# A fused attention and mixture-of-experts kernel: the first expert block outside the loop, expert weights loaded further ahead and split in another order, scatters counted per buffer

## The chip, the cores and the metric

The kernel runs on one core of a Trainium2 chip. The metric is the time of the whole program on the device in microseconds (us). Three runs of the kernel before gave 707.31, 708.02 and 710.58; the median is 708.02. TensorE, VectorE, ScalarE and GpSimd are also written PE, DVE, ACT and POOL; SP is the engine that issues most transfers.

## The reference

Three stages follow one another. The arrays are float32.

```python
# 1: linear attention, B=4, H=8, S=768, D=48
cur = einsum('bhd,bhe->bhde', u[None] * kt, vt)
y[:, :, t] = einsum('bhd,bhde->bhe', rt, state + cur)
state = w[None, :, :, None] * state + einsum('bhd,bhe->bhde', kt, vt)
# 2: dense MLP over 3072 tokens, 384 -> 2048 -> 384
h = x @ w_in
z = maximum(0.01 * h, h) @ w_out
# 3: top-1 mixture of 8 experts (384 -> 1024 -> 384) with a skip score
do_compute = z @ w_skip > 0
e_idx = argmax(z @ w_gate); gate_w = softmax(z @ w_gate)[e_idx]
out = z + gate_w * (maximum(z @ w1[e_idx], 0) @ w2[e_idx])   # only where do_compute
```

## The kernel before, in words

**Everything up to the experts.** Attention runs in 24 chunks of 128 tokens, the MLP in 8 groups of three chunks and 16 steps each, 128 steps in all (STEPS). Every float32 product is made of three float32r products: a value is split into a high part (ScalarE's copy, `_hi`) and a low part (VectorE's difference, `_lo`), and hi·hi, hi·lo and lo·hi are summed. The results z go to `z_rows` in memory and to `out`. Token numbers are scattered by expert into `id_list`, which comes back as `found`; the last group's are placed by TensorE products while the MLP ends (`place_last`, L1405 on). The rows of the first expert block come from two places: `zg_early` (GpSimd's gather, L1758, turned by TensorE, L827) and the last group's rows straight from `z_sb` (L836). Behind L827 TensorE ranks the last group (L751, L753), VectorE's `slot` (L1413) waits for that, and the first block's rows wait for what follows it.

**The expert blocks.** Tokens of one expert are worked on in blocks of 128; a block belongs to one expert. How many blocks there are and which expert each has is known at run time only, in `plan`; TensorE, ScalarE, VectorE and GpSimd each run a loop of eight rounds with four blocks in a round (UNROLL), with a branch around each block, and read from `plan` with register loads (`value_load`). In block j:

- TensorE turns the hidden rows of block j (L855, `hidden_turned`), makes the first product of block j+1 (L816, 18 matmuls, w1), turns the gathered rows of block j+2 (L808, `turn_rows`), and makes the second product of block j (L911, 24 matmuls, w2).
- ScalarE copies the turned hidden rows to `eht_hi` (L1158), and, where block j is the first of its expert e, w2 of expert e+1 to `w2_hi` in three pieces (L1130); then ReLU on the hidden rows of block j+1 (L1137, L1138), `zt_hi` for block j+2 (L1133), and last, where block j+1 is the first of its expert e, w1 of expert e+1 to `w1_hi` in three pieces (L1037).
- VectorE does the low parts in the same order: `eht_lo` (L1634), w2 (L1647), `zt_lo` (L1577), w1 (L1663), and then `res` (L1670), the gate times the second product plus the row itself.
- GpSimd takes the token numbers (`put` L1787, `get` L1792), waits for `res`, gathers the rows of block j+4 (`zg`, four buffers, L1740) and scatters `res` of block j to `out` (L1799). It begins a block only when the scatter of the block before has landed: all scatters count on one semaphore `s_rows_out`. `res` and `put` have two buffers each.

Each engine works through its own list in the order written; the order is set by hand. Raw weights have two places per matrix (expert number even or odd). SP loads them (`load_w1` L521, `load_w2` L529; each is two transfers of 768 KB) and tells ScalarE with `report`. w1 of experts 0 and 1 is loaded and split during the MLP's last group (L1043, L1339), w2 of expert 0 is loaded at the end of the MLP. For each further expert SP waits until the place is free, loads w1, waits again, loads w2, and waits for both to land before it goes on:

```python
report(0)
report(1)
for e in range(2, E):
    if e == 2:
        sp.wait_ge(rows_in[0], 16)
    sp.wait_ge(s_w1_lo, PIECES * (e - 1))
    load_w1(e)
    sp.wait_ge(s_w2_lo, PIECES * (e - 1))
    load_w2(e)
    report(e)
```

Ahead of its loop TensorE makes block 0's first product, turns block 1's rows and block 0's hidden rows, and multiplies out the gate table (`list_gates`, L849).

## Time and profile before

| | |
|---|---|
| time, median of 3 runs | 708.02 us |
| the profiled execution's own time | 704.92 us |
| its span, first to last instruction | 703.0 us |
| mean granted clock of TensorE | 0.992 of full speed |
| TensorE matmuls | 676.8 us busy, 96% of the span |
| VectorE | 411.4 us, 59% |
| ScalarE | 306.6 us, 44% |
| GpSimd | 90.9 us, 13% |
| DMA | 78.04 MB, mean 111 GB/s |
| expert stage in the trace | from about 547 us to 696 us, 14 blocks |

Busy times are of single engines and overlap. In rows of the timeline the first number is the start in us from the span's start, the second how long the row's instructions last; "[1.79 <-issue]" is idle time of that engine just before and what ended it, where "issue" is time in which nothing is seen to be waited for (register loads, branches, dispatch). Starts of neighbouring matmuls overlap by up to 0.25 us, since their ends are modelled. The waits of an engine that is not on the path cost nothing.

### The profile page before, as it was taken

To read this page: it belongs to the slowest core of one execution; us is meant where nothing else is said; L and a number is where in the kernel's file an instruction comes from. 1 tells how busy PE (TensorE), PEld (TensorE's weight loads), DVE (VectorE), ACT (ScalarE), POOL (GpSimd) and SP (SyncE) were. 2 spreads that over 40 slices of the span, in tenths; PEclk is the share of its full clock that TensorE was granted. 3 is DMA by queue.
4 is the path that set the end of the run, shared out by engine and by line. 5 is a ranking of instruction groups with operands and counts; after the bars stand their busy time and mean duration, and the time that the engine had idled before them with its cause. 6 is when DMAs were issued, how large, how long until landed. Compare 5 with 4: busy or idle time off the path is not lost.

```text
span 703.0 us, 14162 instructions
## 1 busy us (share of the span) xinstructions
PE 676.8 (96%) x4374; PEld 643.2 (91%) x4375; DVE 411.4 (59%) x859; ACT 306.6 (44%) x665; POOL 90.9 (13%) x115
## 2 busy tenths in 40 slices
PE   8989999999999999999999999999999889999993
PEld 7989999999999999999999999999998678898883
DVE  8775656655655565556555554633476781573851
ACT  4545435433434443354334344433354362654750
POOL 6530000100010001001000100010020311423411
PEclk9999999999999999999999999999999999999997
DMA  8826624211422132242114222004304586382600
GB/s 242 275 88 202 202 69 136 68 37 38 132 67 69 48 99 62 64 135 68 40 34 132 68 69 73 30 11 168 116 11 159 157 321 233 98 308 74 210 20 8
DMA packets 39081, 78.04 MB, mean 111 GB/s; under 512 B 8578, under 2 KB 27299, under 8 KB 39024
## 3 DMA queue, kind: packets, MB, share of 16 engines
q1 hardware_dynamic: 34064, 62.96, 28.7%
q10 hardware_dynamic: 2432, 9.76, 3.7%
q0 software_dynamic: 2528, 4.60, 2.1%
q8 instruction: 32, 0.52, 0.3%
q14 instruction: 25, 0.20, 0.1%
HBM read 61.29 MB, written 13.00 MB: 106 GB/s over the span
## 4 chain that ended last, share of the span: by engine, by line
PE 83%; DMA 5%; DVE 4%; issue 3%; ACT 1%; DVEq 1%; POOL 1%; ACTq 0%; POOLq 0%; SPq 0%
PE bank L723 29%; PE bank L741 28%; PE bank L816 5%; PE bank L911 5%; PE bank L605 4%; PE bank L661 3%; PE bank L656 3%; PE bank L674 2%; DMA raw<-in_experts 2%; PE bank L699 1%; DMA zg<-z_rows,get 1%; DMA out<-res,put 1%; PE bank L855 1%; PE bank L643 1%; DVE w_lo L1663 1%
## 5 line engine op out<-in xcount | busy, mean ns | idle before, releaser
L1006 ACT ACTIVATE h_sb<-bank 128x384 f32<-128x384 f32 x128 | 62.9, 492 | 246.8 <-PE bank L723 246.8
L1293 DVE TENSOR_TENSOR h_sb<-h_sb,bank 128x384 f32<-128x384 f32 x128 | 70.8, 553 | 169.1 <-ACT h_sb L1006 168.6
L723 PE MATMUL bank<-x_hi,win_hi 128*128 128x384 f32 x384 | 134.7, 351 | 2.0 <-DVE win_lo L1315 1.9
L741 PE MATMUL bank<-wout_hi,g_hi 128*128 128x394 f32 x384 | 132.0, 344 | 0.0
L741 PE MATMUL bank<-wout_hi,g_lo 128*128 128x394 f32 x384 | 131.7, 343 | 0.0
L741 PE MATMUL bank<-wout_lo,g_hi 128*128 128x394 f32 x384 | 131.6, 343 | 0.0
L723 PE MATMUL bank<-x_hi,win_lo 128*128 128x384 f32 x384 | 129.4, 337 | 0.0
L723 PE MATMUL bank<-x_lo,win_hi 128*128 128x384 f32 x384 | 129.3, 337 | 0.0
L1300 DVE TENSOR_TENSOR g_lo<-h_sb,g_hi 128x384 fp32r<-128x384 f32 x128 | 72.0, 563 | 32.7 <-ACT g_hi L1013 31.7
L1013 ACT ACTIVATE g_hi<-h_sb 128x384 fp32r<-128x384 f32 x128 | 66.6, 521 | 43.6 <-DVE h_sb L1293 41.2
L723 PEld LDWEIGHTS bank<-x_hi,win_hi 128*128 128x128 f32 x384 | 72.2, 188 | 8.6 <-issue 6.2
L1705 POOL DMA_INDIRECT id_list<-idgate,dst x21 | 21.3, 1014 | 446.3 <-DVE dst L1398 442.0
L741 PEld LDWEIGHTS bank<-wout_hi,g_lo 128*128 128x128 f32 x384 | 72.8, 190 | 0.0
L741 PEld LDWEIGHTS bank<-wout_lo,g_hi 128*128 128x128 f32 x384 | 72.6, 189 | 0.0
L741 PEld LDWEIGHTS bank<-wout_hi,g_hi 128*128 128x128 f32 x384 | 72.5, 189 | 0.0
L723 PEld LDWEIGHTS bank<-x_lo,win_hi 128*128 128x128 f32 x384 | 72.4, 189 | 0.0
L723 PEld LDWEIGHTS bank<-x_hi,win_lo 128*128 128x128 f32 x384 | 72.2, 188 | 0.0
L963 ACT ACTIVATE am<-const,diag 128x128 f32<-128x128 f32 x168 | 53.2, 391 | 0.0
L911 PE MATMUL bank<-w_hi,eht_hi 128*128 x112 | 38.8, 346 | 3.8 <-DVE eht_lo L1634 3.3
L911 PE MATMUL bank<-w_hi,eht_lo 128*128 x112 | 37.5, 335 | 0.0
L911 PE MATMUL bank<-w_lo,eht_hi 128*128 x112 | 37.5, 335 | 0.0
L1250 DVE COPY_PREDICATED am<-const,bank 128x512 f32<-128x512 uint32 x48 | 32.8, 739 | 2.1 <-PE bank L605 1.4
(217 smaller groups left out, 964.1 us busy)
## 6 DMA issues: line engine op xcount, KB each, us to landing
raw<-in_experts SPq DMA_DIRECT2D x32, 768.0 KB, 6.1
rkt<-in_rk_t SPq DMA_DIRECT2D x46, 192.0 KB, 3.6
rkn<-in_rk_nat SPq DMA_DIRECT2D x21, 384.0 KB, 4.1
z_rows<-z_sb SPq DMA_DIRECT2D x27, 192.0 KB, 2.7
v<-in_v_nat SPq DMA_DIRECT2D x24, 192.0 KB, 2.9
out<-z_sb SPq DMA_DIRECT2D x24, 192.0 KB, 2.8
stage<-in_win ACTq DMA_DIRECT2D x4, 768.0 KB, 4.4
stage<-in_wout_t ACTq DMA_DIRECT2D x4, 768.0 KB, 6.1
```

Source lines behind the costliest of these rows:

```text
L605: mm = pe.matmul(scores_in(n)[q][:, P * p:P * p + P], kb[n % 2][rows, p, :], rt[n % 2][rows, p, :], start=True, stop=True)
L723: mm = pe.matmul(h_ps[t % 2][:, 0:GT], a[:, kk, cols], b[G % 2][:, kk, :], start=n == 0, stop=n == 3 * KT - 1)
L741: mm = pe.matmul(z_ps[i][:, 0:ZW], a[t % 3][:, tok], b[:, f, :], start=f == 0 and j == 0, stop=f == FT - 1 and j == 2)
L816: mm = pe.matmul(eh_ps[c][:], a[par][:, kk, :], b[:, bass.ds(base + EF * kk + 512 * c, 512)], start=kk == 0 and a is zt_hi and b is w1_hi, ...
L911: mm = pe.matmul(ey_ps[u % 2][:, 0:DM], a[:, f, :], b[:, bass.ds(odd * EW + DM * f, DM)], start=f == 0 and a is eht_hi and b is w2_hi, sto ...
L963: ins = act.activation(am_of(n)[h % 2][:, h // 2, :], ident, ACT.Copy, scale=diag_of(n)[:, h:h + 1])
L1006: act.activation(h_sb[t % 2][:], h_ps[t % 2][:, 0:GT], ACT.Copy, scale=SLOPE).then_inc(s_h_scaled, 1)
L1013: act.activation(g_hi[t % 3][:], h_sb[t % 2][:], ACT.Copy).then_inc(s_g_hi_done, 1)
L1250: dve.copy_predicated(am_of(n)[q][:], spread(before.bitcast(U32), 1, [P, PAIRS, P]), scores_in(n)[q][:].rearrange("a (p t) -> a p t", p=PA ...
L1293: dve.tensor_tensor(h_sb[t % 2][:], h_sb[t % 2][:], h_ps[t % 2][:, 0:GT], ALU.max).then_inc(s_leaky, 1)
L1300: dve.tensor_tensor(g_lo[t % 3][:], h_sb[t % 2][:], g_hi[t % 3][:].bitcast(F32), ALU.subtract).then_inc(s_g_lo_done, 1)
L1705: pool.indirect_dma_start(out=id_list[:, :], out_offset=bass.IndirectOffsetOnAxis(ap=dst[:, n:n + 1], axis=0), in_=idgate[:, n, :], in_off ...
```

## The change

1. **TensorE's first block.** The first product of block 1, the turning of block 2's rows and the second product of block 0 stand ahead of the loop, straight behind the gate table; the loop's rounds now hold blocks 1 to 4, 5 to 8 and so on, and the branch for the first round's missing turning is gone. Two register loads (`nxt`, `nxt_odd`) stand ahead of the gate table.
2. **First weights.** w1 of experts 2 and 3 is loaded during the MLP's last group (steps STEPS-6 and STEPS-3), as soon as the place is free. In SP's list behind that, w1 of expert e+1 is now loaded behind w2 of expert e, and the reports for w1 and w2 are apart.
3. **Order of the splits.** On ScalarE and VectorE w1 is split at a block's head, right behind `eht_hi` and `eht_lo`, and w2 at its end. Before it was the other way round.
4. **Scatters.** One semaphore for each of the two `res` buffers: GpSimd begins block j when the scatter of block j-2 has landed.

```diff
@@ -309,7 +309,7 @@
-        s_rows_out = sem("rows_out")
+        rows_out = [sem(f"rows_out{i}") for i in range(2)]
@@ -542,6 +542,10 @@
                     sp.wait_ge(s_scatter, 16 * (TILES - CPG))
                     sp.dma_start(found[:].rearrange("a s x -> a (s x)"),
                                  id_list.rearrange("(p s) x -> p (s x)", p=P)).then_inc(s_found, 16)
+                if step in (STEPS - 6, STEPS - 3):
+                    e = 2 if step == STEPS - 6 else 3
+                    sp.wait_ge(s_w1_lo, PIECES * (e - 1))
+                    load_w1(e)
...
@@ -565,22 +569,30 @@
             sp.wait_ge(rows_in[1], 16)
             load_w2(1)
-            def report(e):
+            def report_w1(e):
                 sp.wait_ge(raw1_load[e % 2], 32 * (e // 2 + 1))
                 sp.sem_inc(s_w1_in, 1)
+
+            def report_w2(e):
                 sp.wait_ge(raw2_load[e % 2], 32 * (e // 2 + 1))
                 sp.sem_inc(s_w2_in, 1)
 
-            report(0)
-            report(1)
+            for e in range(4):
+                report_w1(e)
+            report_w2(0)
+            sp.wait_ge(rows_in[0], 16)
             for e in range(2, E):
-                if e == 2:
-                    sp.wait_ge(rows_in[0], 16)
-                sp.wait_ge(s_w1_lo, PIECES * (e - 1))
-                load_w1(e)
                 sp.wait_ge(s_w2_lo, PIECES * (e - 1))
                 load_w2(e)
-                report(e)
+                if e > 3:
+                    report_w1(e)
+                else:
+                    report_w2(e - 1)
+                if 3 <= e < E - 1:
+                    sp.wait_ge(s_w1_lo, PIECES * e)
+                    load_w1(e + 1)
+                if e >= 3:
+                    report_w2(e)
...
@@ -870,27 +882,42 @@
                 hidden_turned(half)
             pe.wait_ge(s_plan_done, 1)
             blocks = pe.value_load(plan[0:1, TOTAL:TOTAL + 1], min_val=E, max_val=BLOCKS)
+            nxt = pe.value_load(plan[0:1, EXPERT + 1:EXPERT + 2], min_val=0, max_val=E - 1)
+            nxt_odd = pe.value_load(plan[0:1, PARITY + 1:PARITY + 2], min_val=0, max_val=1)
             pe.wait_ge(s_listed, 1)
             list_gates()
+
+            def second_product(par, j, base, pieces):
+                pe.wait_ge(s_w2_lo, pieces)
+                for f in range(EFT):
+                    if f % 4 == 0:
+                        pe.wait_ge(s_eht_lo, 2 * j + f // 4 + 1)
+                    for a, b in ((eht_hi, w2_hi), (eht_hi, w2_lo), (eht_lo, w2_hi)):
+                        mm = pe.matmul(ey_ps[par][:, 0:DM], a[:, f, :], b[:, bass.ds(base + DM * f, DM)],
+                                       start=f == 0 and a is eht_hi and b is w2_hi,
+                                       stop=f == EFT - 1 and a is eht_lo)
+                mm.then_inc(s_ey_done, 1)
+            pe.wait_ge(s_zt_lo, 2)
+            first_product(1, nxt_odd * EW, PIECES * nxt)
+            pe.wait_ge(rows_in[2], 16)
+            turn_rows(2)
+            second_product(0, 0, 0, PIECES)
             with pe.Fori(0, (BLOCKS + 1) // UNROLL) as jj:
-                with pe.If(UNROLL * jj < blocks):
-                    for u in range(UNROLL):
-                        j = UNROLL * jj + u
+                with pe.If(UNROLL * jj + 1 < blocks):
+                    for k in range(UNROLL):
+                        j = UNROLL * jj + 1 + k
+                        u = (1 + k) % UNROLL
...
-                            if u == 0:
-                                with pe.If(jj > 0):
-                                    for half in range(2):
-                                        pe.wait_ge(s_relu_done, 2 * j + half + 1)
-                                        hidden_turned(half)
-                            else:
-                                for half in range(2):
-                                    pe.wait_ge(s_relu_done, 2 * j + half + 1)
-                                    hidden_turned(half)
+                            for half in range(2):
+                                pe.wait_ge(s_relu_done, 2 * j + half + 1)
+                                hidden_turned(half)
...
-                                pe.wait_ge(rows_in[(u + 2) % UNROLL], 16 * (jj + 1 + (u + 2) // UNROLL))
+                                pe.wait_ge(rows_in[(u + 2) % UNROLL], 16 * (jj + 1 + (3 + k) // UNROLL))
                                 turn_rows((u + 2) % UNROLL)
...
-                            mm.then_inc(s_ey_done, 1)
+                            second_product(u % 2, j, odd * EW, PIECES * cur + PIECES)
...
@@ -1158,23 +1176,6 @@
-                            first = act.value_load(plan[0:1, bass.ds(FIRST + j, 1)], min_val=0, max_val=1)
-                            with act.If(first > 0):
-                                e = act.value_load(plan[0:1, bass.ds(EXPERT + j, 1)], min_val=0, max_val=E - 1)
-                                odd = act.value_load(plan[0:1, bass.ds(PARITY + j, 1)], min_val=0, max_val=1)
-                                act.wait_ge(s_w2_in, e + 2)
-
-                                act.wait_ge(s_w2_lo, PIECES * e + PIECES)
-                                high_w2(e + 1, 1 - odd)
-
-                            with act.If(j < blocks - 1):
-                                act.wait_ge(s_eh_done, j + 2)
-                                hidden_rows()
-
-                            with act.If(j < blocks - 2):
-                                act.wait_ge(s_zt_done, j + 3)
-                                turned_rows(u % 2)
-
                             first = act.value_load(plan[0:1, bass.ds(FIRST + j + 1, 1)], min_val=0, max_val=1)
                             with act.If(first > 0):
                                 e = act.value_load(plan[0:1, bass.ds(EXPERT + j + 1, 1)], min_val=0,
@@ -1186,6 +1187,23 @@
                                 act.wait_ge(s_w1_lo, PIECES * e + PIECES)
                                 act.wait_ge(s_eh_done, j + 1)
                                 high_w1(e + 1, 1 - odd)
+                            with act.If(j < blocks - 1):
+                                act.wait_ge(s_eh_done, j + 2)
+                                hidden_rows()
+
+                            with act.If(j < blocks - 2):
+                                act.wait_ge(s_zt_done, j + 3)
+                                turned_rows(u % 2)
+
+                            first = act.value_load(plan[0:1, bass.ds(FIRST + j, 1)], min_val=0, max_val=1)
+                            with act.If(first > 0):
+                                e = act.value_load(plan[0:1, bass.ds(EXPERT + j, 1)], min_val=0, max_val=E - 1)
+                                odd = act.value_load(plan[0:1, bass.ds(PARITY + j, 1)], min_val=0, max_val=1)
+                                act.wait_ge(s_w2_in, e + 2)
+
+                                act.wait_ge(s_w2_lo, PIECES * e + PIECES)
+                                high_w2(e + 1, 1 - odd)
...
@@ -1636,20 +1654,6 @@
-                            first = dve.value_load(plan[0:1, bass.ds(FIRST + j, 1)], min_val=0, max_val=1)
-                            with dve.If(first > 0):
-                                e = dve.value_load(plan[0:1, bass.ds(EXPERT + j, 1)], min_val=0, max_val=E - 1)
-                                odd = dve.value_load(plan[0:1, bass.ds(PARITY + j, 1)], min_val=0, max_val=1)
-                                for i in range(PIECES):
-                                    cols = bass.ds((1 - odd) * EW + PIECE * i, PIECE)
-                                    dve.wait_ge(s_w2_hi, PIECES * e + PIECES + i + 1)
-                                    dve.sem_inc(s_dve_past, 1)
-                                    dve.tensor_tensor(w2_lo[:, cols], raw2[:, cols], w2_hi[:, cols].bitcast(F32),
-                                                      ALU.subtract).then_inc(s_w2_lo, 1)
-
-                            with dve.If(j < blocks - 2):
-                                turned_rows(u % 2, j + 3)
-
                             first = dve.value_load(plan[0:1, bass.ds(FIRST + j + 1, 1)], min_val=0, max_val=1)
                             with dve.If(first > 0):
                                 e = dve.value_load(plan[0:1, bass.ds(EXPERT + j + 1, 1)], min_val=0,
@@ -1662,6 +1666,20 @@
                                     dve.sem_inc(s_dve_past, 1)
                                     dve.tensor_tensor(w1_lo[:, cols], raw1[:, cols], w1_hi[:, cols].bitcast(F32),
                                                       ALU.subtract).then_inc(s_w1_lo, 1)
+                            with dve.If(j < blocks - 2):
+                                turned_rows(u % 2, j + 3)
+
+                            first = dve.value_load(plan[0:1, bass.ds(FIRST + j, 1)], min_val=0, max_val=1)
+                            with dve.If(first > 0):
+                                e = dve.value_load(plan[0:1, bass.ds(EXPERT + j, 1)], min_val=0, max_val=E - 1)
+                                odd = dve.value_load(plan[0:1, bass.ds(PARITY + j, 1)], min_val=0, max_val=1)
+                                for i in range(PIECES):
...
@@ -1780,8 +1798,13 @@
                         j = UNROLL * jj + u
                         with pool.If(j < blocks):
-                            if u > 0:
-                                pool.wait_ge(s_rows_out, 16 * j)
+                            if u < 2:
+                                with pool.If(jj > 0):
+                                    pool.wait_ge(rows_out[u], 32 * jj)
+                                    pool.sem_inc(s_res_free, 1)
+                            else:
+                                pool.wait_ge(rows_out[u % 2], 32 * jj + 16)
                                 pool.sem_inc(s_res_free, 1)
...
@@ -1799,11 +1822,9 @@
-                                oob_is_err=False).then_inc(s_rows_out, 16)
-                            if u == UNROLL - 1:
-                                pool.wait_ge(s_rows_out, 16 * (j + 1))
-                                pool.sem_inc(s_res_free, 1)
-            pool.wait_ge(s_rows_out, 16 * blocks)
+                                oob_is_err=False).then_inc(rows_out[u % 2], 16)
+            pool.wait_ge(rows_out[0], 16 * ((blocks + 1) >> 1))
+            pool.wait_ge(rows_out[1], 16 * (blocks >> 1))
```

The instruction lists show it in two places. SP, from the load of `found` in the MLP's last group on (`raw` is raw1 at L521 and raw2 at L529); lines with + are new:

```order
 L543 DMA found<-id_list 128x384 [waits scatter]
+L521 DMA raw<-in_experts 128x1536 [waits w1_lo]
+L521 DMA raw<-in_experts 128x1536
+L521 DMA raw<-in_experts 128x1536 [waits w1_lo]
+L521 DMA raw<-in_experts 128x1536
 L529 DMA raw<-in_experts 128x1536 [waits h_done]
```

Two loads of w1 have moved ahead of w2 of expert 0, from behind w2 of expert 1, where they waited for four landings. ScalarE, one block of the loop, before:

```order
L1158 ACTIVATE eht_hi<-bank 128x512
...
L1161 TENSOR_LOAD plan
...
L1130 ACTIVATE w_hi<-raw 128x1024
...
L1137 ACTIVATE eh<-bank 128x512
L1138 ACTIVATE eh<-bank 128x512
...
L1133 ACTIVATE zt_hi<-bank 128x384
...
L1178 TENSOR_LOAD plan
...
L1037 ACTIVATE w_hi<-raw 128x1024
```

and the same block of the change (L1055 is the copy of w1, L1148 that of w2):

```order
L1176 ACTIVATE eht_hi<-bank 128x512
...
L1179 TENSOR_LOAD plan
...
L1055 ACTIVATE w_hi<-raw 128x1024
...
L1155 ACTIVATE eh<-bank 128x512
L1156 ACTIVATE eh<-bank 128x512
...
L1151 ACTIVATE zt_hi<-bank 128x384
...
L1199 TENSOR_LOAD plan
...
L1148 ACTIVATE w_hi<-raw 128x1024
```

The two groups of three copies have changed places around ReLU and `zt_hi`; VectorE's list has changed in the same way. TensorE, from the plan's first load to the loop, before:

```order
L872 TENSOR_LOAD plan
L872 ISA x2
L849 MATMUL bank<-gate_col,is_row 128x192 x3
L875 UNCONDITIONAL_BRANCH
L875 ISA
L876 COMPARE_AND_BRANCH
L879 COMPARE_AND_BRANCH
L880 ISA
L880 TENSOR_LOAD plan
```

and of the change (L828 is the first product, L820 the turning of rows, L896 the second product):

```order
L884 TENSOR_LOAD plan
...
L885 TENSOR_LOAD plan
...
L886 TENSOR_LOAD plan
L886 ISA x2
L861 MATMUL bank<-gate_col,is_row 128x192 x3
...
L820 MATMUL bank<-const,zg 128x128 x3
L896 MATMUL bank<-w_hi,eht_hi 128x384
...
L907 UNCONDITIONAL_BRANCH
L907 ISA
L908 COMPARE_AND_BRANCH
```

The loop's entry has moved behind block 0's second product.

## Rows read from the trace of the kernel before

**Rows 1.** The page: the chain that ended last, shares by engine.

```profile
PE 83%; DMA 5%; DVE 4%; issue 3%; ACT 1%; DVEq 1%; POOL 1%; ACTq 0%; POOLq 0%; SPq 0%
```

**Rows 2.** Timeline of TensorE, blocks 0 to 4: start, length, engine, line, tiles, idle before.

```profile
557.08 0.73 PE L816 MATMUL bank<-w_hi,zt_hi 128*128 x2 [1.79 <-issue]
...
561.56 0.42 PE L911 MATMUL bank<-w_hi,eht_hi 128*128 x1
...
573.36 0.44 PE L911 MATMUL bank<-w_hi,eht_hi 128*128 x1 [2.02 <-DVE eht_lo L1634]
...
577.62 0.27 PE L855 MATMUL bank<-const,eh 128*128 128x128 f32 x1
...
593.19 0.33 PE L808 MATMUL bank<-const,zg 128*128 128x128 f32 x1 [0.55 <-DMA zg<-z_rows,get]
...
598.00 0.32 PE L855 MATMUL bank<-const,eh 128*128 128x128 f32 x1
```

**Rows 3.** Timeline of TensorE: starts of first products (L816), and the last second product.

```profile
598.84 0.47 PE L816 MATMUL bank<-w_hi,zt_hi 128*128 x1
...
618.88 0.47 PE L816 MATMUL bank<-w_hi,zt_hi 128*128 x1
...
637.94 0.48 PE L816 MATMUL bank<-w_hi,zt_hi 128*128 x1
...
658.13 0.47 PE L816 MATMUL bank<-w_hi,zt_hi 128*128 x1
...
677.65 0.49 PE L816 MATMUL bank<-w_hi,zt_hi 128*128 x1 [0.21 <-DVE w_lo L1663]
...
689.06 0.44 PE L911 MATMUL bank<-w_hi,eht_hi 128*128 x1 [1.26 <-DVE eht_lo L1634]
```

**Rows 4.** Timeline of ScalarE (three rows), then of VectorE, in expert blocks.

```profile
598.68 1.09 ACT L1158 ACTIVATE eht_hi<-bank 128x512 fp32r<-128x512 f32 x2 [4.41 <-PE bank L855]
...
655.58 2.96 ACT L1037 ACTIVATE w_hi<-raw  x3 [1.26 <-issue]
...
682.60 0.58 ACT L1137 ACTIVATE eh<-bank 128x512 f32<-128x512 f32 x1
...
559.02 1.29 DVE L1634 TENSOR_TENSOR eht_lo<-bank,eht_hi 128x512 fp32r<-128x512 f32 x2 [1.38 <-issue]
...
650.78 1.28 DVE L1634 TENSOR_TENSOR eht_lo<-bank,eht_hi 128x512 fp32r<-128x512 f32 x2
...
657.04 3.50 DVE L1663 TENSOR_TENSOR w_lo<-raw,w_hi  x3 [0.35 <-ACT w_hi L1037]
...
660.99 1.27 DVE L1634 TENSOR_TENSOR eht_lo<-bank,eht_hi 128x512 fp32r<-128x512 f32 x2
...
688.03 1.29 DVE L1634 TENSOR_TENSOR eht_lo<-bank,eht_hi 128x512 fp32r<-128x512 f32 x2 [0.20 <-ACT eht_hi L1158]
```

**Rows 5.** Waits, 530 to 703 us: who waited, for whom, total, times, longest.

```profile
POOL put L1787 <- DMA out<-res,put: 38.7, 10, 7.6
```

**Rows 6.** Timelines of DVE, SP, POOL; DMA issues with us to landing last.

```profile
530.99 1.23 DVE L1339 TENSOR_TENSOR w_lo<-raw,w_hi 128x1024 fp32r<-128x1024 f32 x1 [0.39 <-ACT w_hi L1043]
...
534.55 0.81 SPq L529 DMA_DIRECT2D raw<-in_experts  x2
...
537.78 1.05 POOL L1758 DMA_INDIRECT zg_early<-z_rows,id_early  x1 [20.43 <-DVE id_early L1560]
...
zg_early<-z_rows,id_early POOLq DMA_INDIRECT x1, 3.4
...
542.79 0.18 DVE L1413 TENSOR_TENSOR slot<-bank,pick 128x24 f32<-128x24 f32 x1
...
570.92 0.81 SPq L521 DMA_DIRECT2D raw<-in_experts  x2
...
573.45 0.97 POOL L1740 DMA_INDIRECT zg<-z_rows,get  x1 [12.00 <-DVE res L1670]
...
zg<-z_rows,get POOLq DMA_INDIRECT x1, 7.4
```

14 lines of the change are left out of this document (5 added, 9 removed).

## The prediction

> **What bounds the kernel now.** I first read the page's chain: TensorE holds 83% of the chain that ended last [rows 1], so only its idle places count. All code that changes runs in the last quarter, so I then read TensorE there in the order of time [rows 2]. It is idle at the loop's entry (1.79 before 557.08), before the second product of block 1 (2.02 before 573.36, for VectorE's eht_lo) and before block 5's rows are turned (0.55 before 593.19, for their gather). I number the 14 blocks 0 to 13; experts start at blocks 0, 1, 5, 6, 9, 10, 12 and 13. T is the start of a block's turning of hidden rows (L855).
>
> The starts of the first product [rows 3] give the undisturbed pitch: 618.88 to 637.94 is two blocks, 19.06, so 9.53 each. Everything above it is loss.
>
> **The change, part by part.**
>
> *w1 split at a block's head.* Where an expert has one block only, the next one's w1 came from the tail of a block (4, 8, 11) just ahead of its use. 598.84 to 618.88 is 20.04, a loss of 0.98; 637.94 to 658.13 is 20.19, a loss of 1.13; 658.13 to 677.65 is 19.52, a loss of 0.46, 0.21 of it noted as a wait for w_lo [rows 3]. w_hi now starts right after the block's eht_hi, and w_lo is there 5 us before it is wanted. Behind it ScalarE's ReLU starts up to 0.6 later, and is wanted 3 us later. Term **-2.6**. Ends: -2.6, and -1.1 if the third and one other stay.
>
> *w2 split at the tail.* Seven blocks get a w2 group behind ReLU and zt_hi. Rows 4 show w1 in that same place: ScalarE's w_hi starts 1.26 after zt_hi, at 655.58; VectorE's three pieces take 3.50 from 657.04, and the next eht_lo starts at 660.99, 5.4 behind w_hi; 5.1 where VectorE is free as soon as the first piece (a third of 2.96) is done. TensorE's second product starts 1.03 behind eht_lo (688.03 [rows 4] and 689.06 [rows 3]). In a block with both groups eht_hi ends at T+1.8 (598.68 + 1.09 [rows 4], 598.00 [rows 2]), w1 runs from T+3.0 to 5.9, two ReLUs of 0.58 and zt_hi to 7.3, w2 from 8.5; eht_lo follows at 13.6 to 13.9, the product at 14.6 to 14.9. It is due at 9.5 + 0.8 + 4.5 = 14.8. So blocks 5 and 9 are level: **+0.2**, ends 0 and +1. Blocks 1, 6 and 10, with no w1 in front, have 0.4 to spare. Block 12 has none, since it is followed by the last block, whose second product is already waiting (1.26 before 689.06 [rows 3]). From the last first product's start: 4.4 to its end, 1.1 for ReLU, 1.26, 5.1 and 1.03 make 12.9, against 689.06 - 677.65 = 11.4 before. Term **+1.5**, ends +1.1 and +1.9.
>
> *The first block ahead of the loop.* Two more register loads now stand ahead of the gate products. I price them at 0.5 each, under half of the 1.26 in which ScalarE does three of them with a branch [rows 4]; the 1.79 behind the gate products go. The first product starts near 556.3 instead of 557.08. The rest of the entry (loop, branches, loads) stands behind the 24 matmuls of the second product, which the sequencer can run ahead of; I take 0.3 of it as seen, ends 0 and 1.8.
>
> *First weights one expert further ahead.* In block 0 ScalarE waited for w2 of expert 1 and w1 of expert 2 to land, and VectorE behind it: that made the 2.02 of rows 2. w1 of experts 2 and 3 now lies there, and the work itself is left. By VectorE: eht_lo at 559.02, the next one 10.2 later (650.78 to 660.99, a block with both groups too [rows 4]), and 1.03: 570.3. By TensorE: 556.3 + 9.53 + 4.48 (557.08 to 561.56 [rows 2]) + 0.3, and 0.3 for a gather that is wanted earlier: 570.9. The later one counts, against 573.36 before. Term for entry and block 0 together **-2.5**; ends -1.2 (entry all seen) and -3.0.
>
> *Blocks 2 and 3, and the scatters.* 577.62 to 598.00 is 20.38, 1.32 above two pitches [rows 2]. POOL waited for each scatter to land (38.7 us in ten waits [rows 5]) before it took up the next block, and so gathered late for block 5: 0.55. Counted per buffer, POOL waits for the scatter two blocks back and gathers right behind res. Another 0.3 was zt_lo, queued on VectorE behind w2's split, now ahead of it. The last 0.3 I put down to the loop's back edge, which moves by a block and stays. Term **-1.0**, ends -0.4 and -1.3. In the other blocks POOL has two blocks of TensorE's work as cover, so nothing is won there; POOL's new branch and its second final wait lie in the same cover, and without it would cost under 0.5.
>
> *Two loads moved ahead.* SP issues 1.5 MB for w1(2) near 521, with nothing else under way: nothing. The 1.5 MB for w1(3) wait for the sixth w_lo (530.99 + 1.23 = 532.2) and go out 2.2 ahead of w2(0) at 534.55 [rows 6]; that one waits for nothing new on SP, and lands later for ScalarE, which has 2 us to spare. But zg_early, gathered at 537.78, lands 3.4 later at 541.2; TensorE's ranks come behind it, and at 542.79 VectorE's slot, on which all that follows hangs [rows 6]. How late will it be? A gather at 573.45, 2.5 behind the first of four such loads (570.92), took 7.4: it landed 9.9 behind that first issue. 532.3 + 9.9 = 542.2, one microsecond late. Term **+1.0**; ends 0 (it lands as now) and +4.0 (7.4 from its own issue). I take the value near the low end since the burst is half done when it is issued.
>
> **Sum:** -2.6 + 0.2 + 1.5 - 2.5 - 1.0 + 1.0 = **-3.4 us**. The profiled execution took 704.92 (its span 703.0 and 1.9 around it), 3.1 below the median; I carry the difference over: 708.02 - 3.4 = **704.6**.
>
> **Rivals.**
>
> (a) *The gather is served in turn*, and zg_early is not late. For: it took 3.4 with a pair of loads under way. Against: 7.4 among four. 704.6 - 1.0 = 703.6. The Trainium skill ("DMA: Bandwidth & Descriptors", Queues, rings and completion order) says that each DMA engine takes turns between queues packet by packet, which would give this case; by that rule the 7.4 is not explained, so the trace agrees with it in part.
>
> (b) *The entry's stall only moves*, whole, behind the second product. For: the first execution of the loop's code is still ahead. Against: later block boundaries, with two register loads each, show no idle. Term -1.2 instead of -2.5: 705.9. The Trainium skill ("Runtime: NRT & Kernel Launch", Instruction fetch mechanics) says that a taken branch out of the fetched window stalls until its target is fetched, which speaks for it; no row here tells a fetch from a load.
>
> (c) *zg_early comes 4 us late.* For and against as in the term. 704.6 + 3.0 = 707.6.
>
> (d) *Counting per buffer frees nothing.* The next weights' loads start earlier too and hold the gather for block 5 as before; its 0.55, and 0.3 of the same in a later block, stay: 705.4.
>
> (e) *Slower: the w2 tail.* If in each of the seven tails eht_lo comes x later than I say (register loads, SP's report), TensorE waits 7x less a slack of 0.4 in four of them, 1.6. The gain is gone at x = 0.7; at x = 1.3 it is 9.1 - 1.6 - 3.4 = +4.1: 712.1. For: blocks 5, 9 and 12 have no slack at all. Against: the same place shows 1.26 for the loads.
>
> **How the numbers follow.** The forecast has 0.42, (a) 0.18, (b) 0.11, (c) 0.09, (d) 0.11, (e) 0.09. A measurement of this kernel can tell about 0.5%, 3.5 us, from no change, and the forecast lies at that bound: half of it (0.21), all of (a) and 0.06 of the good ends of (b) and (d) are faster by more, 0.45; (e) is slower, 0.09; 0.46 lies between. The range goes from 702.3, which is (a) with the good ends of entry, blocks 2 and 3, and block 12, to 707.6, which is (c); it leaves out (e) and a little of each side.
>
> **What would show it.** Right: no idle for w_lo ahead of first products; the first product within 0.5 us of the gate products; POOL's gather for block 5 right behind res of block 1; the second product of block 1 near 570.9 plus what zg_early is late; the last second product 12.9 behind the start of the last first product; more idle ahead of L827. Wrong: eht_lo waited for in blocks 2, 6, 7, 10 or 11, which is (e); L827 on time, which is (a); idle of over 1 us behind block 0's second product, which is (b).

## The result: slower by 1.2%, and outside the range

The changed kernel took **718.42 us** (median of 4 runs, 712.39 to 720.71) against 708.17 for the kernel before (707.31 to 710.58): ratio **1.0115**, 95% interval 1.0061 to 1.0168. The quotient of the two medians, 1.0145, lies inside that interval. (Executions of one kernel differ by up to 2.6%, the longer ones at a lower granted clock, and ratios leave out those that are over 1.5% above the kernel's fastest.) The prediction was 704.6 in a range of 702.3 to 707.6, and "slower" had a chance of 0.09. The profiled execution took 720.71, its span is 718.8.

The page of the changed kernel (cut): slices of the span, and the chain that ended last, which answers to [rows 1].

```profile
PE   8989999999999999999999999999998699999983
PEclk9899999999999999999999999999999989999996
...
PE 84%; DVE 4%; issue 3%; DMA 3%; ACT 2%; DVEq 1%; POOL 1%; ACTq 1%; POOLq 0%; SPq 0%
```

The chain looks as before. New are the dips of PEclk in the second slice, in the one at 575 us, and a deeper one in the last. TensorE's own row has a dip too, just ahead of 575.

**Half of the gap between the two profiled executions lies ahead of any changed work.** Busy times and clock by stretch; columns are PE, PEld, DVE, ACT and POOL busy, granted clock, DMA share and GB/s. First the kernel before:

```profile
0.00:50.00 50.00, 44.85 (x359) 42.91 (x361) 41.05 (x91) 23.50 (x61) 26.19 (x34) 1.00 0.70 213
50.00:100.00 50.00, 49.77 (x348) 48.01 (x347) 29.98 (x49) 25.04 (x57) 0.00 (x0) 0.97 0.53 166
...
539.30:703.00 163.70, 144.93 (x786) 126.97 (x784) 93.93 (x162) 77.12 (x116) 41.93 (x58) 0.98 0.46 163
```

The same of the changed kernel:

```profile
0.00:50.00 50.00, 44.58 (x312) 42.74 (x314) 39.27 (x88) 22.79 (x59) 22.52 (x32) 0.90 0.73 212
50.00:100.00 50.00, 49.77 (x337) 48.03 (x337) 29.46 (x46) 22.04 (x50) 2.83 (x3) 0.90 0.43 145
...
548.00:718.80 170.80, 147.89 (x786) 132.03 (x784) 94.01 (x162) 77.56 (x116) 38.30 (x58) 0.95 0.39 141
```

In the first 100 us TensorE is busy for as long, but does 649 matmuls in place of 707: its clock is granted at 0.50 (1.2 GHz) in several stretches, about 20 us in all (the mean of 0.90), where it was 3 to 4 us before. The MLP (the dense two-layer network of the second stage) so ends at 548.05 instead of 539.37, 8.7 us later. The runs below show that this varies by execution: two further kernels with the changed kernel's MLP code end it at 539.30 and 539.79. Whether the change makes it likelier stays open. I therefore compare **the stage from the MLP's last product to the end of the span**: 163.63 us before, **170.75** after. These 7.12 us are the change's, and they are 1.0% of the time. The fastest executions differ by as much: 712.39 among ten of the changed kernel, 705.30 among 29 of the kernel before.

Here is TensorE in the stage; a row is the start, the length, the line and the idle before it:

```profile
551.70 0.94 PE L839 MATMUL bank<-const,zg_early 128*128 128x128 f32 x6 [1.93 <-DMA zg_early<-z_rows,id_early]
...
557.85 0.72 PE L828 MATMUL bank<-w_hi,zt_hi 128*128 128x512 f32 x2 [0.27 <-DVE zt_lo L1595]
...
565.71 1.21 PE L861 MATMUL bank<-gate_col,is_row 128*128 128x192 f32 x6 [1.64 <-issue]
566.63 0.76 PE L828 MATMUL bank<-w_hi,zt_hi 128*128 x2
...
575.19 0.90 PE L820 MATMUL bank<-const,zg 128*128 128x128 f32 x3 [4.14 <-DMA zg<-z_rows,get]
575.74 0.67 PE L896 MATMUL bank<-w_hi,eht_hi 128*128 128x384 f32 x1
576.21 0.52 PE L896 MATMUL bank<-w_lo,eht_hi 128*128 128x384 f32 x1
...
582.12 0.34 PE L896 MATMUL bank<-w_lo,eht_hi 128*128 128x384 f32 x1
```

The forecast did not have the 4.14 at 575.19: the rows of block 2 are not there. Nor did it have what follows. The matmuls of the second product (L896) take 0.52 each from 575.74 to about 581, and 0.34 from then on. POOL had asked for those rows in time, and SP issued two loads of 1.5 MB around that gather, one ahead of it and one behind it. The gather, and in two cuts of SP's queue w2 of expert 1 and w2 of expert 2:

```profile
565.63 2.91 POOL L1758 DMA_INDIRECT zg<-z_rows,get  x1 [0.79 <-POOL get L1764]
```

```profile
562.57 0.81 SPq L529 DMA_DIRECT2D raw<-in_experts  x2
...
567.63 0.80 SPq L529 DMA_DIRECT2D raw<-in_experts  x2
```

The DMA issues of 565.5 to 566 us, with the time to landing last; first the changed kernel, then the same gather in the kernel before (555 to 556 us):

```profile
zg<-z_rows,get POOLq DMA_INDIRECT x1, 9.5
```

```profile
zg<-z_rows,get POOLq DMA_INDIRECT x1, 5.2
```

565.63 + 9.5 = 575.1, which is when TensorE goes on. The kernel before issued its gather at 555.32 and the next loads from 559.29, 4.0 behind it, since its report first waited for w2 of expert 1 to land. Now the last thing that w2 of expert 2 waits for is VectorE's last piece of w2 of expert 0, which frees its buffer, and it goes out 2.0 behind the gather. The 4.14 come out of this. The gather is issued 1.6 later (17.6 instead of 15.9 behind the MLP's end, since zg_early is late) and takes 4.3 longer; against it stand 0.8 by which TensorE wants it later, and 1.0 by which it was early before.

The end of the kernel, TensorE, and then the granted clock by stretch, from block 2's rows to the last product:

```profile
702.36 0.68 PE L896 MATMUL bank<-w_hi,eht_hi 128*128 x1 [3.92 <-DVE eht_lo L1652]
702.84 0.52 PE L896 MATMUL bank<-w_lo,eht_hi 128*128 x1
```

```profile
574.50:581.50 7.00, 6.31 (x22) 6.32 (x23) 3.17 (x5) 3.30 (x4) 0.00 (x0) 0.53 0.04 16
581.50:702.00 120.50, 116.40 (x648) 105.73 (x646) 69.09 (x85) 62.83 (x95) 29.10 (x46) 0.99 0.41 148
702.00:709.50 7.50, 6.74 (x24) 6.42 (x24) 0.79 (x3) 0.00 (x0) 1.36 (x3) 0.64 0.02 7
```

So the granted clock is low in two stretches of the expert blocks, and each belongs to an idle of about 4 us: it falls to 0.50 within the idle and stays there for about 5 to 6 us of the work behind it. The last product's 24 matmuls take 6.7 us instead of 4.4.

In us from the MLP's end (worked out from TensorE's timelines: first and second products of blocks 0, 1 and 13; the tail is from the last second product's start to the end of the span):

```
kernel          MLP end  first 0  first 1  second 0  second 1  first 13  second 13  tail   stage
before           539.37     8.17    17.71     22.19     33.99    138.28     149.69  13.94  163.63
changed          548.05     9.80    18.58     27.69     39.64    140.97     154.31  16.44  170.75
again            544.34    10.81    20.25     28.64     39.72    141.31     154.66  15.70  170.36
hold_w2          545.41     9.70    18.46     23.09     33.02    134.73     148.08  16.41  164.49
fill             539.30     9.62    18.42     28.95     38.49    140.06     153.36  16.94  170.30
cond             541.61     9.69    18.53     27.88     39.73    143.00     154.98  15.71  170.69
hold_last        541.16     9.83    18.63     23.15     33.44    135.63     147.80  15.74  163.54
best             543.38     8.16    16.96     21.69     31.76    134.03     146.33  14.19  160.52
best_inloop      547.87     8.17    17.78     23.85     33.37    135.81     148.03  15.70  163.73
best_onesem      545.81     8.17    16.97     21.45     31.77    134.08     146.53  13.96  160.49
best2            556.55     8.17    17.00     21.65     31.83    133.78     146.49  15.56  162.05
before_again     539.36     8.17    17.72     22.21     34.16    138.14     149.55  13.99  163.54
inloop           539.79     9.70    19.29     27.39     36.91    138.89     152.17  15.74  167.91
w13              542.55     8.17    16.96     26.42     37.11    138.54     151.90  15.75  167.65
```

### The profile page after: what moved, and what is told of

Read it like the earlier page. It is cut to its first block, busy times and chain, and to the rows that moved or that the text cites. A ratio compares the mean times of both kernels' runs of the same rounds, so it can differ in the third digit from the quotient of the medians.

```text
span 718.8 us, 14128 instructions
## 1 busy us (share of the span) xinstructions
PE 688.2 (96%) x4374; PEld 656.5 (91%) x4375; DVE 413.8 (58%) x859; ACT 307.1 (43%) x665; POOL 86.4 (12%) x115
## 4 chain that ended last, share of the span: by engine, by line
PE 84%; DVE 4%; issue 3%; DMA 3%; ACT 2%; DVEq 1%; POOL 1%; ACTq 1%; POOLq 0%; SPq 0%
PE bank L735 29%; PE bank L753 27%; PE bank L896 7%; PE bank L828 5%; PE bank L617 4%; PE bank L673 3%; PE bank L668 3%; PE bank L686 2%; PE bank L711 2%; DMA zg<-z_rows,get 1%; PE bank L867 1%; PE bank L655 1%; DMA zg_early<-z_rows,id_early 1%; DVE h_sb L1311 1%; ACT h_sb L1024 1%
## 5 line engine op out<-in xcount | busy, mean ns | idle before, releaser
L896 PE MATMUL bank<-w_hi,eht_hi 128*128 (+1 forms) x112 | 40.9, 365 | 4.5 <-DVE eht_lo L1652 4.5
L896 PE MATMUL bank<-w_lo,eht_hi 128*128 (+1 forms) x112 | 39.5, 353 | 0.0
L896 PE MATMUL bank<-w_hi,eht_lo 128*128 (+1 forms) x112 | 39.5, 352 | 0.0
L1681 DVE TENSOR_TENSOR w_lo<-raw,w_hi x21 | 24.5, 1220 | 19.2 <-ACT w_hi L1148 19.2
```

The costliest lines, as they stand in the source:

```text
L896: mm = pe.matmul(ey_ps[par][:, 0:DM], a[:, f, :], b[:, bass.ds(base + DM * f, DM)], start=f == 0 and a is eht_hi and b is w2_hi, stop=f == ...
L1681: dve.tensor_tensor(w2_lo[:, cols], raw2[:, cols], w2_hi[:, cols].bitcast(F32), ALU.subtract).then_inc(s_w2_lo, 1)
```

## The experiments

**Theory.** The split reports let SP issue w2 of expert 2 without waiting for w2 of expert 1 to land. This load runs against the gather of block 2's rows, TensorE stands for 4.1 us, and the clock falls behind it. Rivals: TensorE merely reached the place sooner (the first block out of the loop), w1 of expert 3 ahead of w2 of expert 0 is what fills the queues, or the w2 tails are the loss, as rival (e) said. Each ratio is against the kernel before on the same chip; for the first four kernels its median is 708.17 (29 executions, 705.3 to 723.6).

### again: the changed kernel unaltered

> The change itself, unaltered, timed again. Theory: about 8.7 of the 15.8 us of the first profile lie ahead of all changed code, in four stretches of half clock in the first 100 us, and are chance; the change's own share is about +7 (two idles of about 4 us on TensorE and the half clock behind them, less 3.7 won in the steady blocks). So the end of the MLP should lie anywhere between 539 and 548, and the ratio near 1.006 to 1.010. Rival: the early half clock comes with the changed program, and then every run ends the MLP near 548 and the ratio is 1.014 or more.

Measured: 720.39 us, ratio 1.0135 (1.007 to 1.02). The result stands. The MLP ended at 544.34, the stage took 170.36. It is put together in another way, though. The clock fell already behind the idle of 1.74 for zg_early (0.50 from 550 to 553 us) and again from 563 to 566, so TensorE reached block 2's rows later, and its wait there was shorter:

```profile
547.80 0.94 PE L839 MATMUL bank<-const,zg_early 128*128 128x128 f32 x6 [1.74 <-DMA zg_early<-z_rows,id_early]
...
572.67 0.55 PE L820 MATMUL bank<-const,zg 128*128 128x128 f32 x3 [2.72 <-DMA zg<-z_rows,get]
```

### hold_w2: the load of w2 of expert 2 waits for block 2's rows

```diff
             for e in range(4):
...
+                if e == 2:
+                    sp.wait_ge(rows_in[2], 16)
```

> The change, with SP's load of w2(2) held until the rows of block 2 have landed. Theory: the gather for block 2 landed 9.5 us after its issue because the load of w2(2) was issued while it ran; held back, it lands 5 to 5.5 after issue as before, TensorE's 4.1 us of idle ahead of the turned rows shrink to 0.5 or less, the clock behind it stays full (another 2.4 us): 6 to 6.5 us faster than the change. Rival: the gather is late because its descriptors were slow (its issue lasts 2.9 us); then the idle stays above 3 us and the time does not move.

Measured: 713.55 us, ratio 1.0042 (1.0002 to 1.0083). TensorE's waits in the stage, for whom, total, times and longest; in the changed kernel:

```profile
PE bank L896 <- DVE eht_lo L1652: 4.5, 3, 3.9
PE bank L820 <- DMA zg<-z_rows,get: 4.1, 1, 4.1
PE bank L839 <- DMA zg_early<-z_rows,id_early: 1.9, 1, 1.9
```

and with the load held:

```profile
PE bank L898 <- DVE eht_lo L1654: 4.4, 3, 3.9
PE bank L841 <- DMA zg_early<-z_rows,id_early: 1.8, 1, 1.8
PE bank L863 <- issue: 1.6, 1, 1.6
```

The gather's wait is gone and nothing of its size stands in its place. The gather, issued at 562.89, landed after 5.3 us (DMA issues of 562.8 to 563.2 us):

```profile
zg<-z_rows,get POOLq DMA_INDIRECT x1, 5.3
```

The second product of block 0 comes 4.6 earlier, and it runs at full clock, so that block 1's comes 6.6 earlier. The stage falls by 6.26. One added wait on SP takes back most of the loss: the theory stands.

### fill: TensorE kept busy while it waits for those rows

Seven matmuls of constants, whose result nobody reads, stand ahead of the wait.

```diff
             first_product(1, nxt_odd * EW, PIECES * nxt)
+            for i in range(7):
+                pe.matmul(bank[6][:], ident, const[:, 0:4 * P], start=True, stop=True)
             pe.wait_ge(rows_in[2], 16)
```

> The change, with seven matmuls of identity by constants (about 0.6 us each) put into an unused bank between block 0's first product and the wait for block 2's rows, so that TensorE works through the 4.1 us of idle. Theory: the half clock behind the idle is caused by the idle; with it filled the second product of block 0 takes 4.3 instead of 6.7 us: 2.4 faster than the change. Rival: the clock falls for another reason (chance, as in the first 100 us); then the second product still takes 6.7 and nothing is won.

Measured: 717.38 us, ratio 1.0098 (1.0057 to 1.014). The clock behind the wait stays full:

```profile
560.00:575.00 15.00, 15.00 (x66) 10.93 (x65) 7.80 (x9) 6.34 (x9) 1.34 (x3) 1.00 0.35 130
```

Second product to second product takes 9.54 instead of 11.95. So the lost clock is worth 2.4 here, and it hangs on the idle. (That is one profile of each. In again and w13, where the idles were 2.72 and 4.48, the same stretch takes 11.08 and 10.69, so 1.6 and 1.2 were lost.) My filling was too long, though: the second product began 1.26 later (28.95 for 27.69), and the stage won only 0.45.

### cond: w2 at a block's head where the next block needs no w1

```diff
+    own = value_load(FIRST + j)
...
+    with If(own > first):
+        make_w2()      # at the head, as before the change
...
-    with If(own > 0):
+    with If(own + first > 1):
+        make_w2()      # at the tail
```

> The change, but w2 is split at the block's head in blocks that split no w1 (1, 6, 10, 12), and at the tail only where w1 is at the head (0, 5, 9). Theory: block 12's tail made the last second product wait 3.9 us and run at half clock; at the head the wait is about 1.3 again and the clock stays full, 2.6 + 2.4 = 5 faster than the change, with the w1 waits still gone. Rival: the third register load and branch at every block's head (0.5 us on ScalarE and VectorE) make eht_lo late in blocks 6 and 10, and give back 1 or 2 of it.

Measured: 715.17 us, ratio 1.0085 (1.0046 to 1.0125). The last first product to the last second product: 11.98 for 13.34, and the wait for eht_lo falls from 3.9 to 2.5. But the blocks now wait for zt_lo:

```profile
PE bank L820 <- DMA zg<-z_rows,get: 4.4, 1, 4.4
PE bank L828 <- DVE zt_lo L1602: 2.7, 3, 1.3
PE bank L896 <- DVE eht_lo L1659: 2.5, 1, 2.5
```

The stage is level (170.69), and the expected 5 us did not come. The last wait was to be 1.3 with a full clock behind it; at 2.5 the clock still fell (tail 15.71). What the end won, blocks 6 and 10 gave back, as the rival had it, though by zt_lo and not by eht_lo. The w2 tail is right in the middle of the run and wrong only at its end. Rival (e), a loss in all seven tails, falls: in the changed kernel the blocks from first product 5 to 13 take 77.25 (611.77 to 689.02), before 78.81 [rows 3], and 79.17 in cond.

### hold_last: hold_w2, and w2 at the head in the last blocks only

```diff
+    with If(j > blocks - 3):
+        ...            # w2 at the head
     with If(j < blocks - 2):
         ...            # zt of block j + 3, then w2 at the tail
```

(The second condition was there, around zt alone.)

> As hold_w2, and in the last two blocks alone w2 is split ahead of ReLU (in the run cond this was done in four blocks, and blocks 6 and 10 then waited 1.3 and 1.1 us for zt_lo). Theory: the wait before the last second product falls from 3.9 to about 1.3 us, no half clock follows it, and from the last first product's start to the last second product's start it is 11.4 or less instead of 13.3; no wait for zt_lo in blocks 6 and 10. Rival: the half clock at the end comes whatever the wait is; then the last second product still takes over 6 us.

Measured in one run: 706.49, stage 163.54. The last wait is 2.73, and the last second product starts 12.17 behind the last first product. Both fall short of the expectation (1.3, and 11.4 or less), and the last second product took 6.0, near the rival's number, so half clock was still there. What did go are the waits for zt_lo in blocks 6 and 10: at most 0.4 is left.

### best: hold_last, and w1 of expert 3 not ahead of w2 of expert 0

```diff
-                if step in (STEPS - 6, STEPS - 3):
-                    e = 2 if step == STEPS - 6 else 3
-                    sp.wait_ge(s_w1_lo, PIECES * (e - 1))
-                    load_w1(e)
+                if step == STEPS - 6:
+                    sp.wait_ge(s_w1_lo, PIECES)
+                    load_w1(2)
...
+                if e == 2:
+                    sp.wait_ge(s_w1_lo, PIECES * 2)
+                    load_w1(3)      # behind load_w2(2)
```

> As hold_last, and w1(3) is not loaded ahead of w2(0) but behind w2(2). Theory: zg_early lands 3.4 us after its issue again instead of 4.2, TensorE's idle ahead of L839/L841 is about 1.0 instead of 1.8, and the whole is below the kernel before: from the end of the MLP's last product to the end of the span 159 to 160 us against 163.6 before, so a ratio of about 0.995. Rival: w1(3) now collides with a gather of the first blocks (block 3's rows), and a wait of 1 us or more stands ahead of L820 there.

Measured: **705.67 us** (702.52 to 708.78, 12 runs), ratio **0.9957** (0.9926 to 0.9988) against 708.03 on its chip. It is faster than both kernels. TensorE's waits:

```profile
PE bank L902 <- DVE eht_lo L1668: 3.2, 2, 2.9
PE bank L867 <- issue: 1.7, 1, 1.7
PE bank L834 <- DVE zt_lo L1611: 1.0, 3, 0.4
PE bank L854 <- DVE is_first L1455: 0.7, 1, 0.7
PE bank L826 <- DMA zg<-z_rows,id_next: 0.3, 1, 0.3
```

zg_early is on time, the first product comes 8.16 behind the MLP as before the change, and the stage is 160.52, 3.1 below before's. The expected 159 to 160 was missed by half a microsecond; the rival's wait of 1 us or more is 0.3. Part of the gain is luck: the last wait is 2.85, hardly more than hold_last's, yet the clock stayed full in this execution (tail 14.19 instead of 15.74). (The expectation gave zg_early's landing as 4.2 in the changed kernel; the row there says 5.2, and the table below uses that.)

### best_inloop and best_onesem: two parts undone in best

The first puts TensorE's block 0 back into the loop, the second counts the scatters on one semaphore again.

> As best, with TensorE's first block back in the loop as before. Theory: 1.8 us of issue idle stand again behind the gate products, but these start 1.3 earlier without the two register loads; so the first product of block 1 starts only 0.5 later than in best, and the end 0 to 0.5 later. Rival: the first block ahead of the loop is worth the 1.8 us in full.

> As best, with all scatters on one semaphore as before. Theory: POOL waits for each scatter to land, the gather for block 5 is issued later than right behind res, but 0.55 us of TensorE's idle come back only if it lands behind a load of weights; from 0 to 0.7 us slower than best. Rival: nothing changes on TensorE, since the loads that were in the way lie elsewhere now.

Measured, one run each. **best_inloop**: 713.42, stage 163.73. The first product of block 1 comes 0.82 later, and part of it is at half clock (a mean of 0.79 from 564 to 572 us), behind an idle of 1.87. Another 1.5 of the 3.2 is the clock at the end, which fell behind a last wait of 2.80 (tail 15.70). So the stage lost more than the expected 0 to 0.5, but most of the excess is clock that fell here and not in best, and one run of each can't tell chance from the entry's idle. **best_onesem**: 708.14, but stage 160.49 against 160.52. As far as one profile can show, counting per buffer is worth nothing once the loads are in order.

### best2: best without one question in block 12

Whether w1 is to be made is not asked in the last but one block.

```diff
+    with If(j < blocks - 2):
         first = value_load(FIRST + j + 1)
         with If(first > 0):
             ...        # w1, as it was
```

> The kernel of the run before it that was fastest (load of w2(2) held until the gather for block 2 has landed, w2 split at the head only in the last block, w1(3) not ahead of w2(0)), and in addition the question about w1 at the head is not asked any more in block 12, so ScalarE and VectorE load one register fewer there. Theory A, the last wait of TensorE (2.9 us before the last second product) contains those register loads: it falls to about 2.2 us, the start of the last second product stands at 11.7 instead of 12.3 us behind the last first product, the stage behind the MLP is 159.3 to 160.2 us instead of 160.5, and the time is 0.5% to 0.7% below before's. Theory B, the register loads lie beside other work: wait, stage (160.5) and ratio (0.996) stay as they were.

Measured: 711.54 us (12 runs, 705.09 to 720.56) against 710.23, ratio 0.9963 (0.9921 to 1.0005): no difference from best that can be told. In the trace ScalarE does begin 0.6 earlier behind eht_hi (idle 1.97 instead of 2.56), but VectorE doesn't follow:

```profile
693.28 1.29 DVE L1669 TENSOR_TENSOR eht_lo<-bank,eht_hi 128x512 fp32r<-128x512 f32 x2 [2.68 <-issue]
698.17 3.49 DVE L1697 TENSOR_TENSOR w_lo<-raw,w_hi  x3 [3.60 <-issue]
701.58 0.61 DVE L1718 SCALAR_TENSOR_TENSOR res<-bank,found,zg 128x384 f32<-128x384 f32 x1
702.11 1.27 DVE L1669 TENSOR_TENSOR eht_lo<-bank,eht_hi 128x512 fp32r<-128x512 f32 x2
```

It starts its three pieces 3.60 behind eht_lo with nobody to wait for (in best 2.95, and there for ScalarE); w_hi's three pieces on ScalarE were done at 696.03. The last wait of TensorE grew from 2.85 to 3.30. Theory A had the wrong engine, by this one trace. What VectorE does in those 3.6 us (the branch runs there for the first time) no row tells.

### before_again: the kernel before, unaltered

> The kernel before, unaltered. Theory A, the half-clock stretches of the first 100 us come by chance in any kernel: the MLP's last product ends anywhere from 539 to 548 us, and the stage behind it is 163.6 us whatever that end was. Theory B, they belong to the change: the MLP ends at 539 to 540 us again.

Measured: 704.79, MLP's end 539.36, stage 163.54. Taken alone it is B. The other kernels decide: the MLP's part is the same in all of them but for the moved load of w1, and it ended at 539.30 in fill, 539.79 in inloop, 541.61 in cond, 548.05 in the changed kernel and 556.55 in best2. In that last one TensorE had the clock at 0.50 from about 11 to 47 us, while it was busy throughout:

```profile
12.00:16.00 4.00, 4.00 (x27) 3.55 (x26) 1.55 (x3) 0.52 (x2) 1.73 (x2) 0.50 1.08 387
...
40.00:44.00 4.00, 4.00 (x16) 4.00 (x15) 1.23 (x3) 2.21 (x3) 0.00 (x0) 0.50 0.21 18
44.00:48.00 4.00, 4.00 (x20) 4.00 (x20) 3.11 (x5) 1.27 (x4) 0.00 (x0) 0.57 0.47 182
```

Two executions of the same changed kernel ended the MLP at 548.05 and 544.34, and the kernel before itself ran from 705.3 to 723.6. So the early stretches vary by execution, and they don't come with the change every time. Whether the change makes them likelier isn't settled: both profiles of before have only 3 to 4 us of them. The kernel before does lose clock in other executions, for its mean granted clock ran from 0.992 (705.30 us) down to 0.963 (723.60 us) among 29; where it lost it, no trace shows.

### inloop and w13: two parts undone in the changed kernel

inloop puts TensorE's block 0 back into the loop, w13 moves w1 of expert 3 behind w2 of expert 2.

> The changed kernel with TensorE's first block put back into the loop, everything else kept. Theory A, the load of w2(2) that is issued behind the gather for block 2 delays that gather: TensorE's wait before the gathered rows of block 2 are transposed stays at 3.3 us or more (4.1 in the changed kernel), and the half clock behind it stays too. Theory B, the wait is there because TensorE is ahead by the first block out of the loop: it falls by the whole 0.8 us that the first product came earlier and by the 1.9 us of idle before the gated rows, to under 2.5 us.

> The changed kernel with one edit: the first weights of block 3 are issued behind the second weights of block 2, no longer ahead of those of block 0. Theory A, these two loads ahead of the gathered rows delay the gated rows: the first product of block 0 comes 8.2 us behind the MLP's end, as before, in place of 9.8, while the wait of about 4 us for the gather of block 2 stays. Theory B, the gated rows wait for something else: 9.6 us or more. The stage by A: 169.0 to 169.6 us (170.75 in the changed kernel).

**inloop**: 709.59, stage 167.91. The wait fell to 1.92. By its number that is theory B (under 2.5), and it is below A's. The rows say why:

```profile
559.08 1.22 PE L828 MATMUL bank<-w_hi,zt_hi 128*128 x2 [1.79 <-issue]
560.09 1.05 PE L828 MATMUL bank<-w_lo,zt_hi 128*128 x2
...
564.34 0.62 PE L828 MATMUL bank<-w_hi,zt_lo 128*128 x2
566.88 0.55 PE L820 MATMUL bank<-const,zg 128*128 128x128 f32 x3 [1.92 <-DMA zg<-z_rows,get]
```

The clock now falls behind the 1.79 at the entry, so block 1's first product takes 5.9 instead of 4.4, and starts 0.7 later. Both eat the wait: 4.14 - 0.7 - 1.5 = 1.9. The rows themselves come when they did: 566.88 is 27.09 behind the MLP's end, and 575.19 in the changed kernel is 27.14. So the gather is late whatever TensorE does, as A says, but A's price of the wait was wrong. Since the half clock was spent beneath the wait, none came behind it; block 1's second product comes 2.7 earlier, and the stage is 2.8 shorter.

**w13**: 712.07, stage 167.65. The first product of block 0 comes 8.17 behind the MLP, as A said, and the wait for the gather is 4.48. That gather was issued at 558.50, 2.0 ahead of w2 of expert 2 (560.49), and landed 0.4 behind it, though w2 of expert 1, issued before it, had landed at 561.6. The issues of 560.4 to 562 us, then of 558.4 to 559:

```profile
raw<-in_experts SPq DMA_DIRECT2D x2, 768.0 KB, 7.5
...
zg<-z_rows,get POOLq DMA_INDIRECT x1, 9.9
```

So w1 of expert 3 is what delays zg_early, and isn't what delays block 2's rows. The stage came out 1.4 to 2.0 below A's numbers, since less was at half clock: block 0's second product to block 1's took 10.69 instead of 11.95, and the tail 15.75 instead of 16.44.

## Why the prediction was wrong

By its own terms, in us; measured in the changed kernel by the table of stages and TensorE's starts.

```
term (or its absence)                         forecast   measured
zg_early behind w1(3)                           +1.0      +1.6
entry of the loop                               -0.8      -0.8
w1 at the head, waits for w_lo                  -2.6      -2.6
w2 tails in blocks 5 and 9                      +0.2      +1.0
blocks 2 and 3                                  -1.0      -1.3
last block                                      +1.5      +1.9
block 0's wait for eht_lo                       -2.3      -2.3
rest of the entry, behind block 0               +0.3       0.0
gather for block 2 against the load of w2(2)    +0.3      +4.6
half clock behind that wait                      -        +2.4
half clock behind the last wait                  -        +2.5
```

The rows of the right column add up to 7.0, against 7.12 in the stage; the left one to the forecast's -3.4, whose -2.5 for entry and block 0 is the -0.8, -2.3, +0.3 and +0.3 of the table. The right column is one execution: in again the parts are others (first product of block 0 at 10.81, wait for block 2's rows 2.72) and the stage is nearly the same.

**The step that failed is "0.3 for a gather that is wanted earlier".** I listed the two loads of w1 that the change moves, and stopped. The split report moves a third, of w2 of expert 2: from 4.8 behind that gather's issue to 2.0 behind it. I even had the price in [rows 6], where a gather beside four such loads took 7.4, and used it for zg_early only. That zg_early is late adds nothing to this wait: in w13 it is on time, and the wait is 4.48.

**A term was missing: what an idle of TensorE costs beyond itself.** In the changed kernel's profile each wait of 4 us came with 2.4 or 2.5 more at 1.2 GHz, once in block 0 and once at the end. Behind idles of 3.9 to 4.5 in the other executions it was 1.2 to 2.3 in block 0 (w13, cond) and 1.8 to 3.0 at the end. fill shows the first directly. The second is in the tail: 13.9 to 14.2 in before, before_again, best and best_onesem, whose last idle was 1.3, 2.9 or 3.0, and 15.6 to 16.9 in all others, with 2.5 to 3.9. So with last idles from 2.5 to 3.3 both occurred, and with 3.9 the clock fell every time (six executions of five kernels). The forecast counted waits at their length alone. Without the two clock terms and the gather's 4.6 the right column adds up to -2.5.

**The last block** was the right mechanism, slightly too cheap: +1.9 instead of +1.5, the upper end. 13.34 from first product to second instead of 12.9. **Blocks 5 and 9**: the starts at 640.86 and 679.51 come 10.02 and 10.05 behind the ones before them, 0.5 each above the pitch of 9.53; the forecast held them level and gave +1 as the far end. This is the sign that was named for (e), eht_lo waited for in blocks 6 and 10, at 0.25 and 0.28 us; blocks 2, 7 and 11 have none of it, so two tails were misjudged and not seven.

**zg_early**: the value near the low end was chosen "since the burst is half done". It landed 5.2 behind its issue, 1.8 more than in [rows 6], and the forecast had 4.4. Rival (a), by which zg_early is not late, is refuted. The rule beside it, that each DMA engine takes turns between queues (the Trainium skill, "DMA: Bandwidth & Descriptors", Queues, rings and completion order), did not give the time here; whether turns are taken no run tests. In w13 a gather landed with the load that was issued 2.0 behind it. The same section says that a semaphore increment lands only after every earlier write of that DMA engine, across its queues. That fits the gathers here; no run separates the two.

**What was right**: waits for w_lo are gone in all blocks; entry; blocks 2 and 3; and, once the load is held (hold_w2), the second product of block 1 comes at 33.02 although zg_early is 1.5 late, 31.8 where it isn't (best); the forecast was 570.9 - 539.37 = 31.5. Rival (b), the entry's stall only moves, did not happen: behind block 0's second product no idle is seen (block 1's comes 9.54 later in fill, a whole pitch). What is left of the entry is 1.64 of "issue" ahead of the gate products (L861), where there were 0.32 ahead of them and 1.79 behind them. Rival (d) is half right: counting per buffer frees nothing in best_onesem, while the 1.3 of blocks 2 and 3 came anyway. No run separates the place of zt_lo from the order of the loads there.

Do the stages explain the measured medians? Ratio times 708.2, minus 708.2, beside the stage's difference to before: changed +8.1 and +7.1, again +9.6 and +6.7, hold_w2 +3.0 and +0.9, fill +6.9 and +6.7, cond +6.0 and +7.1, best -3.0 and -3.1, best2 -2.6 and -1.6. The two agree within the intervals, which reach 2 to 4.6 us to either side, while a stage is one execution.

## What to carry to other kernels

When a report or a semaphore is split, list every transfer that can start earlier by it, also those of code that the change leaves as it was, and look for a small gather that is wanted within the next 10 us; one wait of the loading queue for that gather recovered 6.3 us here. Price an idle of 4 us on TensorE at 5 to 7, the half clock behind it included (1.2 to 3.0 in these traces). Work that is moved to the tail of a block to get out of the way is right in the steady state and wrong in the block ahead of the last: give that one its old order.

## What the hardware did that I had not expected

- A gather of 128 rows landed 9.5, 9.6 and 9.9 us after its issue where 1.5 MB of weights were asked for 2.0 us behind it (changed kernel, inloop, w13), just behind those weights in the last two; it took 5.2 or 5.3 where the next load came 4.0 or 5.4 behind it (before, hold_w2).
- TensorE's granted clock was 0.50 for 5.9 us of work behind an idle of 4.1, in a kernel that had kept it busy for 90% or more of every slice of the page from 54 to 539 us. It also fell behind idles of 1.74 (again), 1.79 (inloop) and 1.87 (best_inloop), where it stayed at 1.0 behind 1.79 in the kernel before and 1.67 in best.
- In the first 100 us half clock came while TensorE was fully busy, for 3 to 4 us in one execution (before) and for 36 in another (best2): 539.3 to 556.6 for the same work.
- In best2 VectorE stood for 3.60 us in "issue" at a branch that it took for the first time.
